# Four first attention chunks with inputs and an order of work of their own, and layer 2 inside both branches, in a fused attention and two-layer kernel

## The reference

```python
for t in range(S):
    cur = np.einsum('bhd,bhe->bhde', u[None] * kt, vt)
    y[:, :, t] = np.einsum('bhd,bhde->bhe', rt, state + cur)
    state = w[None, :, :, None] * state + np.einsum('bhd,bhe->bhde', kt, vt)
x = (x @ w_a) * (x @ w_b) @ w_out            # layer 1, inner width 1536
h = x @ w_in                                 # layer 2, inner width 2048
g = h * np.clip(h + 3.0, 0.0, 6.0) / 6.0
return g @ w_out
```

## Time and profile before

| | before |
|---|---|
| median of 3 runs | 972.81 us |
| profiled execution | 973.0 us |
| its span, first to last instruction | 971.2 us |
| outside the span | 1.8 us |
| PE busy | 935.7 us (96%) |
| DVE, ACT, POOL busy | 369.1, 328.7, 183.9 us |
| granted TensorE clock, mean | 0.977 |

### The profile page before, as it was taken

How to read it: one execution, slowest core, us unless ns; L and a number is a source line. 1 busy time by engine, 2 the same in 40 slices (tenths; PEclk the granted TensorE clock), 3 DMA queues, 4 the chain that set the end, 5 groups by cost and what they waited for, 6 DMA issues and landing times.

```text
span 971.2 us, 13219 instructions
## 1 busy us (share of the span) xinstructions
PE 935.7 (96%) x5478; PEld 763.1 (79%) x5478; DVE 369.1 (38%) x588; ACT 328.7 (34%) x641; POOL 183.9 (19%) x162
## 2 busy tenths in 40 slices
PE   5479999999999999999999989999999999999998
PEld 3358888888888888888788868888888888888887
DVE  5345533442444334333322234334334343343332
ACT  2444432323323323323222233333333343333333
POOL 5547520121011111101065574000000000000000
PEclk7579999999999999999999999999999999999999
DMA  5444320312112113113031221010010100100000
GB/s 178 143 141 147 120 68 33 99 50 82 49 50 81 51 50 98 50 50 114 1 122 50 58 84 49 1 66 1 23 42 1 33 33 1 65 1 1 33 1 32
DMA packets 22757, 57.09 MB, mean 59 GB/s; under 512 B 2209, under 2 KB 6178, under 8 KB 22690
## 3 DMA queue, kind: packets, MB, share of 16 engines
q1 hardware_dynamic: 18290, 47.52, 15.3%
q10 hardware_dynamic: 4400, 8.65, 2.3%
HBM read 46.73 MB, written 9.44 MB: 58 GB/s over the span
## 4 chain that ended last, share of the span: by engine, by line
PE 94%; DMA 3%; DVE 1%; issue 1%; ACT 0%; SPq 0%; POOL 0%; ACTq 0%; DVEq 0%
PE up_ps L502 31%; PE up_ps L565 20%; PE acc_ps L516 15%; PE att_ps L579 10%; PE acc_ps L579 10%; PE att_ps L437 3%; PE att_ps L452 1%; PE att_ps L473 1%; PE att_ps L478 1%; DMA rkT<-in_rk_turned 1%; DMA causal_sb<-in_causal 1%; PE att_ps L468 1%; DMA w_raw<-in_moe_w_out 1%; DVE rkT L758 1%; PE att_ps L462 1%
## 5 line engine op out<-in xcount | busy, mean ns | idle before, releaser
L502 PE MATMUL up_ps<-x_cut,w_up 128*128 128x512 f32 x1296 | 312.2, 395 | 7.3 <-DVE x_cut L800 7.0
L502 PEld LDWEIGHTS up_ps<-x_cut,w_up 128*128 128x128 f32 x1296 | 242.7, 189 | 62.4 <-DVE x_cut L800 7.3
L673 ACT ACTIVATE g_cut<-tmp 128x512 fp32r<-128x512 f32 x168 | 106.2, 632 | 217.3 <-DVE tmp L843 144.6
L851 DVE SCALAR_TENSOR_TENSOR g_cut<-tmp,g_cut 128x512 fp32r<-128x512 f32 x168 | 123.6, 735 | 117.3 <-ACT g_cut L673 117.3
L516 PE MATMUL acc_ps<-g_cut,w_down 128*128 128x512 f32 x648 | 158.0, 391 | 0.0
L516 PEld LDWEIGHTS acc_ps<-g_cut,w_down 128*128 128x128 f32 x648 | 120.9, 188 | 26.3 <-issue 1.0
L845 DVE SCALAR_TENSOR_TENSOR tmp<-tmp,up_ps 128x512 f32<-128x512 f32 x96 | 66.1, 688 | 188.0 <-ACT tmp L667 188.0
L667 ACT ACTIVATE tmp<-up_ps,three 128x512 f32<-128x512 f32 x96 | 66.2, 690 | 176.4 <-PE up_ps L565 171.9
L843 DVE TENSOR_TENSOR tmp<-tmp,up_ps 128x512 f32<-128x512 f32 x72 | 49.5, 687 | 192.3 <-PE up_ps L502 187.2
L565 PE MATMUL up_ps<-x_cut,w_in_first 128*128 128x512 f32 x432 | 107.2, 393 | 3.4 <-DVE tmp L845 3.4
L565 PE MATMUL up_ps<-x_cut,w_up 128*128 128x512 f32 x432 | 105.7, 389 | 0.0
(11 more groups left out here) (78 smaller groups left out, 555.6 us busy)
## 6 DMA issues: line engine op xcount, KB each, us to landing
nat<-in_natural SPq DMA_DIRECT2D x24, 704.0 KB, 5.7
rkT<-in_rk_turned SPq DMA_DIRECT2D x24, 448.0 KB, 3.9
w_raw<-in_moe_w_out SPq DMA_DIRECT2D x28, 192.0 KB, 2.3
layer_out_T<-stage ACTq DMA_DIRECT2D x6, 768.0 KB, 3.3
x_cut<-layer_out_T SPq DMA_DIRECT2D x6, 768.0 KB, 4.3
outT<-stage ACTq DMA_DIRECT2D x5, 768.0 KB, 3.3
w_raw<-in_moe_w_in SPq DMA_DIRECT2D x12, 256.0 KB, 3.2
w_raw<-in_moe_w_a SPq DMA_DIRECT2D x9, 256.0 KB, 8.0
```

What stands on the lines that cost most here:

```text
L502: mm = pe.matmul(up_ps[:, m, :], w_up[:, a, m, c, cols], x_cut[:, t % 2, b, c, :], start=(c == 0 and z == 0), stop=(c == KC - 1 and z == 2))
L673: nc.scalar.activation(g_cut[:, n % GR, HI, :], tmp[:, n % 2, :], ACT.Copy, scale=1.0 if n < TILES * N1 else 1.0 / 6.0).then_inc(s_gh, 1)
L851: dve.scalar_tensor_tensor(out=lo, in0=tmp[:, n % 2, :], scalar=1.0 if n < TILES * N1 else 1.0 / 6.0, in1=hi.bitcast(F32), op0=ALU.mult, o ...
```

## The change

The order of the kernel's parts stays; eight things change.

1. The first four chunks get buffers of their own, `first_rk`, `first_k` and `first_v` (no r by step), and `prod`. They lie where `w_down` lies later. SP loads all of them without waiting for a `y`; `u_all` (192 KB) goes from the first transfers to later ones.
2. Their own weights are made by `first_product` (POOL, one product of r and k, 112x512) and `own_of_first` (PE, four products with 2 moving columns), copied by ACT to `own_first`.
3. Their additions to the state (`decayed_keys` on POOL, `increment` on PE) come after the four outputs, all four before layer 1.
4. EARLY is 6: pieces 6 and up, the first that are written over the chunks' buffers, are cut in slots; ACT enters layer 1 only when the additions are made.
5. On POOL the six `cut_low` stand ahead of the four `decayed_keys`; the state's memset stands behind the products.
6. ACT makes own weights and diagonals of chunks 0 and 1 ahead of the first cuts and of `tab_s`.
7. DVE does not wait for the constants ahead of the first `scale`, and no `own_weight` stands between the first chunks.
8. Layer 2 is written inside `If` and inside `Else`, on all five engines.

```diff
-EARLY = 8
+EARLY = 6
+            first_rk = sb("first_rk", [P, B, 2, NP, CH], of=prologue, align=ALIGN)
+            first_k = sb("first_k", [P, B, H * D], of=prologue)
+            first_v = sb("first_v", [P, B, H * D + H * EM], of=prologue)
+            prod = sb("prod", [P, 2, NP, CH], of=prologue)
         w_down = sb("w_down", [P, 2, N1, DM], F32R, align=ALIGN)
...
+        def first_product(pool, q):
+            pool.wait_ge(s_frk[q], 16)
+            if q >= 2:
+                pool.wait_ge(s_own_ps, q - 1)
+            nc.gpsimd.tensor_tensor(out=prod[0:W2, q % 2], in0=rk_at(q)[0:W2, 0], in1=rk_at(q)[0:W2, 1],
+                                    op=ALU.mult).then_inc(s_prod, 1)
...
+        def own_of_first(pe, q):
+            pe.wait_ge(s_prod, q + 1)
+            pe.wait_ge(s_u, 16)
+            if q >= 2:
+                pe.wait_ge(s_own_first, q - 1)
+            for p in range(NP):
+                mm = pe.matmul(own_ps(q)[:, 2 * p:2 * p + 2], prod[0:W2, q % 2, p, :], u_col[0:W2, p, :],
+                               start=True, stop=True, skip_group_check=True)
+            mm.then_inc(s_own_ps, 1)
+        def increment(pe, q):
+            pe.wait_ge(s_kh, q + 1)
...
         def sync_fast(sp):
-            for m in range(STAGES):
-                load_piece(sp, m)
+            load_piece(sp, 0)
+            load_first_v(sp, 1)
+            load_first_rk(sp, 3)
+            load_piece(sp, 1)
+            load_first_v(sp, 2)
+            load_piece(sp, 2)
+            load_first_v(sp, 3)
+            load_first_k(sp, 0)
+            load_first_k(sp, 1)
             load_piece(sp, 3)
+            load_first_k(sp, 2)
+            load_first_k(sp, 3)
             load_piece(sp, 4)
...
+            sp.dma_start(u_all[:], u.unsqueeze(0).to_broadcast([P, H, D])).then_inc(s_u, 16)
+            load_natural(sp, B)
+            load_piece(sp, 5)
+            load_rk(sp, B)
...
+            sync_layer2(sp)
         def scalar_fast(act):
+            act.wait_ge(s_ident, 16)
+            def own_and_diagonal(q):
+                act.wait_ge(s_own_ps, q + 1)
+                nc.scalar.activation(own_first[:, q], own_ps(q), ACT.Copy).then_inc(s_own_first, 1)
+                for half in range(2):
+                    diagonal(act, q, half)
...
+            own_and_diagonal(3)
+            x_high(act, 1, True)
+            cut_high(act, 3)
+            x_high(act, 2, True)
+            cut_high(act, 4)
+            x_high(act, 3, True)
+            cut_high(act, 5)
+            act.wait_ge(s_delta, B)
             scalar_layer1(act, True)
+            scalar_layer2(act)
```

More of the change, by code:

```diff
@@ L452, in outputs @@
                     pe.matmul(y_ps[part:part + HP, place(p // 2)], state[0:W2, q % B, p, 0:2 * EM],
[L453 to L464 removed]
+                              rk_at(q)[0:W2, 0, p, :], start=(p < 2), stop=False, skip_group_check=True)
+            v_loaded(pe, q)
+            if earlier and has_state(q):
+                increment(pe, q)
             if earlier:
@@ L551, in tensor_fast @@
             outputs(pe, 3)
+            for q in range(B):
+                increment(pe, q)
             tensor_layer1(pe, True)
+            tensor_layer2(pe)
         def up2(pe, t, i):
@@ L606, in diagonal @@
             if half == 0:
-                act.wait_ge(s_own, q + 1)
+                if q < B:
+                    act.wait_ge(s_own_first, q + 1)
+                else:
+                    act.wait_ge(s_own, q - B + 1)
                 if q >= 2:
                     act.wait_ge(s_y, q - 1)
+            mine = own_first[:, q] if q < B else own[:, q % 2]
             for p in range(NP):
                 h = 2 * p + half
-                ins = nc.scalar.activation(A[:, q % 2, half, p, :], id_sb[:], ACT.Copy, scale=own[:, q % 2, h:h + 1])
+                ins = nc.scalar.activation(A[:, q % 2, half, p, :], id_sb[:], ACT.Copy, scale=mine[:, h:h + 1])
             ins.then_inc(s_diag, 1)
@@ L728, in scalar_fast @@
         def scalar_fast(act):
+            act.wait_ge(s_ident, 16)
+            def own_and_diagonal(q):
+                act.wait_ge(s_own_ps, q + 1)
+                nc.scalar.activation(own_first[:, q], own_ps(q), ACT.Copy).then_inc(s_own_first, 1)
+                for half in range(2):
+                    diagonal(act, q, half)
+            own_and_diagonal(0)
+            own_and_diagonal(1)
+            cut_high(act, 0)
+            cut_high(act, 1)
             act.wait_ge(s_tab_ps, 1)
@@ L733, in scalar_fast @@
                                ACT.Copy).then_inc(s_tab, 1)
[L734 to L742 removed]
+            own_and_diagonal(2)
+            x_high(act, 0, True)
+            cut_high(act, 2)
+            own_and_diagonal(3)
[6 more added lines that the diff above has]
+            act.wait_ge(s_delta, B)
             scalar_layer1(act, True)
+            scalar_layer2(act)
         def scalar_general(act):
```

176 lines of the change are left out of this document (101 added, 75 removed).

## The result

| | before | after |
|---|---|---|
| median | 972.18 us (4 runs, 971.41 to 973.5) | 957.11 us (4 runs, 956.61 to 958.47) |
| profiled execution, its span | 973.0, 971.2 us | 956.6, 954.8 us |
| granted TensorE clock, mean | 0.977 | 0.986 |

The ratio is 0.9846, 95% interval 0.9829 to 0.9863: the kernel became 15 us faster. The forecast was 955.6, and all but 0.6 us of the difference of the spans lies at the three places it named.

What follows compares the result with a forecast made beforehand. PE bounds the kernel, with time to win in the first 60 us, through late transfers, and where the layers meet. 973.0 - 14.0 (start) - 4.9 (meeting) + 1.5 (end) = 955.6 us, range 950.5 to 961.

Steps and rivals of the forecast that it cites:

- The start of layer 1: First chunks, before layer 1: layer 1 starts at 40.0 instead of 54.0, 14.0 us less, released by POOL's keys and PE's additions.
- rivals A and B: Start: A, PE at full clock, layer 1 at 33.5, 949.1, chance 0.08; B, POOL and transfers slower, 960, chance 0.16.
- own products: Start, on PE: four products with 2 moving columns for each chunk's own weight, taken at 1.0 us.
- last outputs: Start, on PE: the outputs of chunk 3, taken at 1.9 us, ending at 32.3.
- Rival E: Start: slower than before, if the fourth r and k transfer lands at 34.5 or later; 975.5 for 37; chance 0.03.
- Tile 0: Layer 1's first tile: pieces 8 to 13 come two slots later; charged 0, with 2 us as the other end.
- The meeting of the layers: Between layers 1 and 2: 4.9 us go without the branch, some 3.4 of waiting and 1.5 of fallen clock.
- Rival C: Between the layers: the gap stays, from ACT's other function or its store, not the branch; 959.0; chance 0.07.
- The end of the program: Behind layer 2: engines now jump over the longer `Else`, SP waits for ACT; 1.5 us more, ends 0 and 3.9.
- Rival D: End of the program: the jump is paid by SP as well, or whole behind ACT's; 958.0; chance 0.08.

Runs made afterwards that it cites:

- double_own: The changed kernel with the four products of each chunk's own weight made twice (the same result); 962.07 us, ratio 0.9901.
- ring_order: ring_waits with one change: on DVE the scaling of chunk 2 stands behind the mask of chunk 1 instead of ahead of it; 966.03 us, ratio 0.9951.
- keys_early: The changed kernel with POOL's four `decayed_keys` moved forward, three behind the second `cut_low` and one behind the third; 952.67 us, ratio 0.9806.
- join_all: The changed kernel with layer 2 written once again behind both branches on all five engines, the new start kept; 958.37 us, ratio 0.9863.
- before_early6: The kernel before with EARLY = 6 alone, so pieces 6 and 7 are not cut ahead of layer 1; 966.86 us, ratio 0.9949.
- ring_waits: The changed kernel with loads of chunks 2 and 3 waiting for y of chunks 0 and 1, their own products behind the first two outputs; 971.64 us, ratio 0.9995.
- join_sp: The changed kernel with layer 2 behind both branches on SP alone, the other four engines keeping it inside; 955.68 us, ratio 0.9834.

## Why the prediction was right

**The start of layer 1**: 39.4 for 40.0, -14.6 for -14.0. The path was the one foretold link by link, down to POOL's keys, and rivals A and B did not come about: the clock was half from 16 to 24 us, and no load on this path was late. The single steps were off in both directions. The own products were taken at 1.0 us and are 1.86 at 18.70 and 1.5 of the path at 15.23; double_own (4.25 later for 3.4 more of them) agrees with all of it being on the path. Against this, the last outputs took 1.1 instead of 1.9 (31.24 to 32.33), since the clock had risen again by 28 us, and the steps of ACT and DVE ahead of them some 0.3 less than taken. The first outputs end at 22.4 for 21.4, and where piece 5's `cut_low` starts the errors have cancelled (33.46 for 33.4). The right sum owes something to that.

**What the prediction did not divide.** It took the start as one. The runs divide it: 7.2 us of the way are EARLY = 6 alone, and with the waits of shared buffers, in the one good order tried (ring_order), no more than about that is had.

**Rival E** was far off: POOL's product of the fourth r and k, which had waited for that transfer, starts at 16.03, not at the 34.5 from which the rival would have decided.

**Tile 0**: charged 0. No stall at block 4; between the start of layer 1 and the meeting it is 0.6 us less than before. The slow clock at its start was foretold as unchanged; keys_early shows 2 us in it that could be had.

**The meeting of the layers**: -5.2 for -4.9. Rival C (the gap stays) is refuted by ACT's 0.52, and by join_all, where it returns with the branch. The working gave 1.5 of it to a fallen clock. In join_all, with the same 4.4 us on ACT, it is 10.0 us from layer 2's first product to the group behind (556.09 to 566.11), where it was 11.3 before, so this share seems to differ. It is only later: in join_all the group of L666 itself takes 3.27 us, and in the kernel before 2.24. One group further, at 569.22 in join_all and here before,

```profile
584.44 2.20 PE L565 MATMUL up_ps<-x_cut,w_in_first 128*128 128x512 f32 x9
```

it is 13.1 and 13.4 us.

**The end of the program** is the term that was mis-sized: +4.0 for +1.5. The prediction's step was that "SP, whose last transfer lands with the span's end at 971.2, waits 1.5" for ACT, with SP's own jump free. Both halves of the step failed. ACT's jump is waited for by nobody: ACT arrives at 950.7, 1.3 us ahead of SP's branch. And SP's own jump is not free: it costs 2.3. The rest, 1.6, is in no term of the sum and in no rival: the last transfer lands after 3.6 us instead of 2.0. Rival D (SP pays too, 3.9 in all) came nearest, and its price fits by luck, as a sum of two other amounts; the larger gains at the two other places covered the miss.

The Trainium skill ("Runtime: NRT & Kernel Launch", Instruction fetch mechanics) has the stall for a taken branch whose target is outside of the blocks at hand. The runs agree in kind: 44 instructions skipped cost SP 0.2 us at most, 243 cost it 2.5, and ACT's passage at the meeting costs 3.9.

## What to carry to other kernels

A branch over long code cost its engine 2.5 us (SP, at the end) to 3.9 us (ACT, at the meeting), and beside such jumps a last transfer landed 1.6 us later. Moving a branch away from a busy place only pays if it lands in a wait, and the end of the program is no such place. Before inputs are given buffers of their own, look at how many of the steps ahead of the first big product need to be there at all, and at which waiting instruction stands ahead of ready ones on another engine: here the one was worth 5.6 us (before_early6) and the other 5.6 (ring_order against ring_waits), beside some 9 for the buffers. The gap of PE just before its long work cost its length here, and then 2 us more in clock. To find what an end of a program waits for, look when each engine arrives there: here the arithmetic fitted ACT within 0.25 us, and the trace says that it was the transfer.

## What the runs showed of the hardware

- Four fp32 products with 2 moving columns (eight records) take 0.95 us at the full clock and 1.86 us at 1.2 GHz. Four of `weights`, with 128 columns and 48 rows in place of 112, take 1.04 at 1.2 GHz (half of 2.08). So the few columns save nothing; per product these took even longer, though with 112 rows for 48, which no run separates. The row at the full clock, from the change:

```profile
8.05 0.95 PE L517 MATMUL acc_ps<-u_col,prod 112*128 112x2 f32 x8
```

- The row of ACT's table load names no operand, but it ran only when PE's own products had ended ACT's first wait, after 9 us of idle time. Its 1.28 us lie ahead of the diagonals of chunk 0, which had time here:

```profile
9.09 1.28 ACT L829 ACT_TABLE_LOAD   x1 [9.09 <-PE acc_ps L517]
```

- The clock does not come back at once with the work: in the change it was granted 0.55 from 40 to 44 us, although PE was busy all of that stretch and had been for 3.8 of the 4 us before, after a gap of 3.4 us.
- A jump at the end of the program over 243 instructions held SP for 2.5 us, over 44 for 0.2; and the 256 KB in flight beside the other engines' jumps took 3.6 to 4.1 us instead of 2.0 (join_sp, above).
